# Pooled attention and two MLPs on one core: a reordered end of batch 0, with half weight splits and an earlier third f-block

## What is computed

```python
def _attn_ref(q, k, v):
    k_p = k.reshape(B, H, Sp, 8, D).mean(axis=3)        # Sp = 72 pooled positions
    v_p = v.reshape(B, H, Sp, 8, D).mean(axis=3)
    scores = scale * np.matmul(q, k_p.transpose(0, 1, 3, 2))
    scores = scores - np.max(scores, axis=-1, keepdims=True)
    attn = np.exp(scores)
    attn = attn / (np.sum(attn, axis=-1, keepdims=True) + 1e-09)
    return np.matmul(attn, v_p)

def _moe_ref(x, w_in, w_out):          # x: attention output, heads side by side
    h = np.maximum(x @ w_in, 0.0)
    return h * h @ w_out

def _moe2_ref(x, w_in, w_out):
    h = x @ w_in
    g = np.where(h >= 1, h, np.where(h <= -1, 0.0, (h + 1) ** 2 / 4))
    return g @ w_out
```

## Time and profile before

| | |
|---|---|
| median of 3 runs | 1772.68 us (1771.05 to 1774.06) |
| profiled execution | 1771.15 us |
| its span, first to last instruction | 1769.4 us |
| TensorE busy | 1751.3 us, 99% |
| VectorE, ScalarE, GpSimd busy | 761.8, 553.7, 229.7 us |
| first `output(0)` begins at | 49.12 us |
| mean granted TensorE clock | 0.996 of full speed |

### The profile page before, as it was taken

The page is one execution under the profiler, slowest core; times in us unless marked ns, Lnnn a source line. Parts: engine busy times, 40 slices in busy tenths (PEclk is TensorE's granted clock), DMA queues, the critical chain, the costliest instruction groups (busy, mean ns, idle before and its releaser), DMA issues.

```text
span 1769.4 us, 22412 instructions
## 1 busy us (share of the span) xinstructions
PE 1751.3 (99%) x8371; PEld 1413.9 (80%) x8371; DVE 761.8 (43%) x1211; ACT 553.7 (31%) x970; POOL 229.7 (13%) x254
## 2 busy tenths in 40 slices
PE   8999999999999999999999999999999999999999
PEld 6777777777777777778888788888888888888887
DVE  6664434444444443433235434343434343434343
ACT  5453333333333333332234322222222222222222
POOL 6332313223131231310000000000000000000000
PEclk8999999999999999999999999999999999999999
DMA  6453324242331423213035202020201020201000
GB/s 153 126 153 122 85 71 120 65 124 81 104 99 59 130 74 118 84 61 107 1 116 170 95 1 72 1 71 0 71 0 71 0 71 0 71 0 71 0 24 24
DMA packets 117062, 126.86 MB, mean 72 GB/s; under 512 B 40192, under 2 KB 72448, under 8 KB 116992
## 3 DMA queue, kind: packets, MB, share of 16 engines
q1 hardware_dynamic: 116992, 125.86, 23.1%
HBM read 80.74 MB, written 45.09 MB: 71 GB/s over the span
## 4 chain that ended last, share of the span: by engine, by line
PE 96%; DVE 2%; ACT 1%; issue 0%; DMA 0%; POOL 0%; SPq 0%; ACTq 0%
PE ps_h L931 44%; PE ps_y L968 44%; PE ps_a L882 2%; PE ps_a L906 2%; PE ps_a L919 2%; PE ps_a L896 1%; DVE sq_f L726 1%; DMA first_kv<-in_v 0%; PE ps_h L941 0%; ACT act_f L569 0%; PE ps_y L863 0%; PE ps_y L852 0%; DVE probs L664 0%; DVE stat L662 0%; POOL first_kv L434 0%
## 5 line engine op out<-in xcount | busy, mean ns | idle before, releaser
L931 PE MATMUL ps_h<-xc,w_hi 128*128 128x512 f32 x2288 | 715.1, 394 | 0.0
L931 PEld LDWEIGHTS ps_h<-xc,w_hi 128*128 128x128 f32 x2288 | 423.0, 188 | 93.4 <-issue 9.2
L931 PE MATMUL ps_h<-xc,w_lo 128*128 128x512 f32 x1144 | 446.7, 390 | 0.0
L968 PE MATMUL ps_y<-w_hi,g_hl 128*128 128x512 f32 x1152 | 379.6, 391 | 3.1 <-DVE stage L750 2.2
L968 PE MATMUL ps_y<-g_hl,w_hi 128*128 128x512 f32 x1152 | 366.3, 399 | 1.5 <-DVE g_hl L730 1.5
L726 DVE TENSOR_TENSOR sq_f<-act_f 128x512 f32<-128x512 f32 x144 | 111.4, 774 | 414.0 <-ACT act_f L569 414.0
L968 PEld LDWEIGHTS ps_y<-w_hi,g_hl 128*128 128x128 f32 x1152 | 217.1, 188 | 49.0 <-DVE stage L750 2.6
L968 PEld LDWEIGHTS ps_y<-g_hl,w_hi 128*128 128x128 f32 x1152 | 209.7, 188 | 57.2 <-issue 15.3
L576 ACT ACTIVATE act_f<-act_f,half_bias 128x512 f32<-128x512 f32 x144 | 104.2, 724 | 480.2 <-DVE act_f L737 480.2
L931 PEld LDWEIGHTS ps_h<-xc,w_lo 128*128 128x128 f32 x1144 | 214.5, 188 | 46.4
L968 PE MATMUL ps_y<-g_hl,w_lo 128*128 128x512 f32 x576 | 225.7, 392 | 0.0
(11 more groups left out here) (81 smaller groups left out, 945.9 us busy)
## 6 DMA issues: line engine op xcount, KB each, us to landing
mlp_out_hl<-stage SPq DMA_DIRECT2D x36, 512.0 KB, 4.3
xc<-mlp_out_hl SPq DMA_DIRECT2D x36, 512.0 KB, 5.7
xc<-attn_out_hl SPq DMA_DIRECT2D x32, 512.0 KB, 3.9
attn_out_hl<-xo_hl SPq DMA_DIRECT2D x56, 288.0 KB, 2.3
out<-stage SPq DMA_DIRECT2D x36, 256.0 KB, 2.1
stage<-in_moe_w_in SPq DMA_DIRECT2D x32, 256.0 KB, 3.6
stage<-in_moe_w_out SPq DMA_DIRECT2D x32, 256.0 KB, 4.7
kv_raw<-in_k SPq DMA_DIRECT2D x28, 288.0 KB
```

Of the source, the lines that this page charges most:

```text
L931: mm = nc.tensor.matmul(ps_h[:, f % 2, :], left[:, f, kd * P:(kd + 1) * P], xc[:, buf, right, kd, :], start=(kd == 0 and n == 0), stop=(kd ...
L968: mm = nc.tensor.matmul(ps_y[:, m, :], left, right, start=(f == 0 and n == 0), stop=(f == NF - 1 and n == 2))
```

## The change

Nothing that is computed for the output changes but the place of the factor 1/8 of the mean over v.

- **Large matmuls in front of the value matmuls.** `first_hidden_hi(0)` and `(1)` move ahead of `first_pv(5)` and `first_pv(6)`; the low-weight matmuls of k-blocks 0 and 1 move ahead of `first_pv(7)`. Within a piece the products with x high come first, and the last k-block waits for `x_hi_done` before `x_split`.
- **Half weight splits.** Blocks 0 and 1 are split in halves of 512 columns: ScalarE splits the first halves in units 6 and 7 and the second halves after the last `first_x_hi`; GpSimd makes four half low parts in place of two whole ones. `output(0)` and `output(1)` wait for the second halves. Block 2 is no longer split before the MLP begins: its split on ScalarE and its low part on VectorE stand behind those engines' work on f-blocks 0 and 1.
- **Column-stepped transposes.** `first_turn_p` writes every third column of PSUM, so that `first_copy_p` copies contiguously, with the factor 1/8.
- **A two-tile addition.** Adding 1e-9 was one operation with two constants (add, times 8); it is now the sum of two SBUF tiles, `stat` and `eps_t`.
- **Third f-block at once.** `hidden(2)` of chunk 0 comes before `output(0)`, behind a wait for `relu_done`.
- Also: k is loaded before q, and k is pooled before q is turned for unit 0; GpSimd's sums of v lie more between the scalings; `first_x_lo(4)` to `(7)` all come after `last_scale`; three more matmuls of `keep_warm`.

```diff
@@ SyncE
-                    sp.wait_ge(w_first, n - 3)
+                    sp.wait_ge(w_first, n - 1)
+            first_load_k(0)
             first_load_q(0)
-            first_load_k(0)
@@ GpSimd
-            def first_w_lo(n):
-                pool.wait_ge(w_hi_done, n + 1)
-                nc.gpsimd.tensor_tensor(w_lo[:, n, :], stage[:, n, :], w_hi[:, n, :].bitcast(F32),
+            def first_w_lo(n, half):
+                part = slice(half * DM, (half + 1) * DM)
+                pool.wait_ge(w_first_hi, 2 * half + n + 1)
+                nc.gpsimd.tensor_tensor(w_lo[:, n, part], stage[:, n, part], w_hi[:, n, part].bitcast(F32),
                                         ALU.subtract).then_inc(w_first, 1)
             first_scale(6)
-            first_w_lo(0)
-            first_w_lo(1)
+            for half in range(2):
+                for n in range(2):
+                    first_w_lo(n, half)
@@ ScalarE
+            def first_split_w(n, half):
+                part = slice(half * DM, (half + 1) * DM)
+                act.wait_ge(w_loaded[n], 2 * DMA)
+                nc.scalar.copy(w_hi[:, n, part], stage[:, n, part]).then_inc(w_first_hi, 1)
-                nc.scalar.copy(p_t[:].rearrange("n a (p j) -> n a j p", j=NJ),
-                               ps_y[0:SP_, 0:2, 0:HALF].rearrange("n a (j p) -> n a j p", j=NJ)).then_inc(p_copied, 1)
+                nc.scalar.activation(p_t[:], ps_y[0:SP_, 0:2, 0:HALF], ACT.Copy, scale=1.0 / POOL).then_inc(p_copied, 1)
@@ in chunk(), ScalarE and VectorE
+                    if layer == 1 and c.at(0) and f == 0:
+                        split_w(2)
                     if layer == 1 and c.at(0) and f + 3 < NF:
                         split_w(f + 3)
@@ ScalarE, in the loop over units and behind it
-                if u >= 5:
-                    split_w(u - 5)
+                if u >= NU - 2:
+                    first_split_w(u - NU + 2, 0)
             first_x_hi(NU - 1)
+            for n in range(2):
+                first_split_w(n, 1)
@@ VectorE
-                nc.vector.tensor_scalar(stat[:, u % 2, 2, :], stat[:, u % 2, 1, :], EPS, float(POOL),
-                                        ALU.add, ALU.mult).then_inc(eps_done, 1)
+                nc.vector.tensor_tensor(stat[:, u % 2, 2, :], stat[:, u % 2, 1, :], eps_t[:],
+                                        ALU.add).then_inc(eps_done, 1)
-                if u >= 3:
+                if 3 <= u < NU - 1:
                     first_x_lo(u - 3)
             first_sums(NU - 1)
             last_scale()
-            first_x_lo(NU - 3)
-            first_x_lo(NU - 2)
-            split_w(2)
-            first_x_lo(NU - 1)
+            for u in range(NU - 4, NU):
+                first_x_lo(u)
@@ TensorE
-                        mm = nc.tensor.transpose(ps_y[0:SP_, a, j * QT:(j + 1) * QT],
+                        mm = nc.tensor.transpose(ps_y[0:SP_, a, 0:HALF].rearrange("n (p j) -> n j p", j=NJ)[:, j, :],
+                if c.at(0) and f < 2:
+                    pe.wait_ge(w_first, f + 3)
                 pe.wait_ge(g_ready, c.times(NF, f + 1))
-                    if f + 2 < NF:
+                    if fixed == 0 and f == 0:
+                        pass
+                    elif f + 2 < NF:
...
+            pe.wait_ge(relu_done, 1)
+            hidden(At(0), 0, 2, 0)
             chunk(At(0), 0, True, 1)
```

More of the change, by code:

```diff
@@ L823, in first_turn_q, with first_pool_k @@
                 mm.then_inc(q_turned, 1)
-                if u % 2 == 0:
-                    pe.wait_ge(k_first[u // 2], DMA)
-                    for e in range(POOL):
-                        for a in range(2):
-                            mm = nc.tensor.matmul(first_q_bank(u + 1)[a * D:(a + 1) * D, HALF:HALF + SP_],
-                                                  first_k[:, u // 2, a, e * D:(e + 1) * D], ident[0:SP_, 0:SP_],
-                                                  start=(e == 0), stop=(e == POOL - 1))
-                    mm.then_inc(k_turned, 1)
+            def first_pool_k(hp):
+                pe.wait_ge(k_first[hp], DMA)
+                for e in range(POOL):
+                    for a in range(2):
+                        mm = nc.tensor.matmul(first_q_bank(1)[a * D:(a + 1) * D, HALF:HALF + SP_],
+                                              first_k[:, hp, a, e * D:(e + 1) * D], ident[0:SP_, 0:SP_],
+                                              start=(e == 0), stop=(e == POOL - 1))
+                mm.then_inc(k_turned, 1)
             def first_scores(u):
@@ L934, in hidden, with first_hidden @@
                 mm.then_inc(h_ready, 1)
-            def first_hidden_hi(f, blocks):
-                pe.wait_ge(w_hi_done, f + 1)
-                for kd in blocks:
-                    pe.wait_ge(x_split, 2 * kd + 2)
-                    for right in range(2):
-                        nc.tensor.matmul(ps_h[:, f, :], w_hi[:, f, kd * P:(kd + 1) * P], xc[:, 0, right, kd, :],
-                                         start=(kd == 0 and right == 0), stop=False)
+            def first_hidden(f, left, right, blocks, start=False, stop=False):
+                for kd in blocks:
+                    mm = nc.tensor.matmul(ps_h[:, f, :], left[:, f, kd * P:(kd + 1) * P], xc[:, 0, right, kd, :],
+                                          start=(start and kd == blocks[0]), stop=stop)
+                if stop:
+                    mm.then_inc(h_ready, 1)
+            def first_hidden_hi(f, blocks):
+                pe.wait_ge(w_first_hi, f + 1)
+                pe.wait_ge(x_split, 2 * blocks[-1] + 2)
+                first_hidden(f, w_hi, 0, blocks, start=(0 in blocks))
+                first_hidden(f, w_hi, 1, blocks)
             def first_hidden_lo(f, blocks):
                 pe.wait_ge(w_first, f + 1)
-                for kd in blocks:
-                    mm = nc.tensor.matmul(ps_h[:, f, :], w_lo[:, f, kd * P:(kd + 1) * P], xc[:, 0, 0, kd, :],
-                                          start=False, stop=(kd == KD - 1))
-                if KD - 1 in blocks:
-                    mm.then_inc(h_ready, 1)
+                first_hidden(f, w_lo, 0, blocks)
             def output(c, f, layer):
+                if c.at(0) and f < 2:
+                    pe.wait_ge(w_first, f + 3)
                 pe.wait_ge(g_ready, c.times(NF, f + 1))
@@ L992, in _ @@
             pe.wait_ge(consts_ready, 1)
+            first_pool_k(0)
             first_turn_q(0)
-            keep_warm(2)
+            keep_warm(3)
             first_scores(0)
             first_turn_q(1)
-            keep_warm(1)
+            keep_warm(2)
             for u in range(NU - 1):
@@ L1001, in _ @@
                     first_turn_q(u + 2)
+                if u % 2 == 0 and u + 2 < NU:
+                    first_pool_k(u // 2 + 1)
                 if u < 2:
-                    keep_warm(2)
+                    keep_warm(2 + u)
                 if u >= 2:
```

54 lines of the change are left out of this document (34 added, 20 removed).

## The result

The changed kernel takes 1775.88 us (median of 20 runs, 1772.77 to 1779.11), the kernel before, run beside it, 1771.19 us (20 runs, 1767.01 to 1774.25). The ratio of the runs is 1.0029, with a 95% interval of 1.0021 to 1.0036: slower by 0.29%, some 5 us (4.7 us between the medians). The profiled execution spans 1773.4 us, 4.0 more than before. The time lies in my range, but on its slower side: the forecast "within 0.2%" was wrong. Now and then an execution of any of these kernels runs at a lower clock throughout (1929.57 us in experiment 9, 2179.91 us in experiment 10); the ratios leave such executions out, the medians given for these two experiments take one in each.

A forecast was written before the change was run, and what follows sets the result against it. TensorE was taken as the bound (96% of the chain of waits), with the dense f-block stream's start deciding. Terms -1.8 - 6.6 + 6.3 + 0.85 + 1.8 = +0.55 us gave a median of 1773.2 us, range 1767.5 to 1777.0.

The forecast's parts named there:

- within 0.2%: Whole kernel: a difference under 0.2%, 3.5 us, was to be called no change; this outcome was given 0.54.
- A: Start of batch 0: GpSimd's scaling behind the first v pair alone, k pooled before q; turn at 14.85, -1.8 us.
- B: Last units: shorter splits and copy, large matmuls filling a wait, addition not shut out; first relu at 40.4, -6.6 us.
- R: The start of the first relu, from which the prediction counts times at the start of the MLP.
- C: Start of the MLP: `hidden(2)` waits for block 2's late low part, VectorE taking turns with GpSimd; +6.3 us.
- D: Batch 1's first scores: they follow the turn of q at once and wait for copies of q and k; +0.85 us.
- E: `hidden(2)` and `output(0)`: after TensorE idles about 7.5 us, their first 3.6 us run at half rate; +1.8 us.
- they get in at the next gap: Last units: two-input VectorE operations enter between GpSimd operations, so the addition of unit 7 ends at 33.5.
- third rival: Last units: the two-tile addition waits for both GpSimd half parts, 2.4 us late; sum +2.1, 1774.8 us; chance 0.10.
- second rival: Last units: the clock falls anyway, the path doubles from about 34 on; sum +4.5, 1777.2 us; chance 0.15.
- first rival: Start of the MLP: VectorE largely free of GpSimd, `hidden(2)` wait only +2.6; 1769.6 to 1767.7 us; chance 0.33.
- the sign that I had named for rivals 2 and 3: End of the last units: a first relu after 41 us, where the forecast had it near 38.6.

The follow-up runs named there:

- experiment 9: The kernel before, with GpSimd starting its two whole low weight parts only after VectorE has scaled unit 7: 1770.02 us, ratio 0.9988.
- experiment 10: The changed kernel with GpSimd's order of v sums and scalings as before (both pairs of v summed ahead of the first scaling): 1778.31 us, ratio 1.0036.
- experiment 7: The changed kernel with block 2 split before the MLP, GpSimd's low parts held until VectorE's last scaling, k sums before second half low parts: 1763.35 us, ratio 0.9961.
- Experiment 6: The changed kernel with block 2 split before the MLP and GpSimd's first half low parts held until VectorE's last scaling: 1763.87 us, ratio 0.9965.
- Experiment 4: The changed kernel with GpSimd waiting for VectorE's last scaling before its first half low parts: 1772.27 us, ratio 1.0014.
- Experiment 3: The changed kernel with GpSimd's k sums of batch 1 put before its second half low parts: 1776.08 us, ratio 1.0039.
- experiment 1: The changed kernel with the third f-block, `hidden(2)`, put back behind `output(0)`: 1769.52 us, ratio 1.0000.
- experiment 2: The changed kernel with weight block 2 split before the MLP begins, as before: 1767.12 us, ratio 0.9989.
- experiment 5: The changed kernel with the addition of 1e-9 as one operation with two constants (add, times 1): 1776.14 us, ratio 1.0036.
- experiment 8: The kernel before with only the third f-block at once, `hidden(2)` in front of `output(0)`: 1771.52 us, ratio 0.9999.

## Why the prediction was right, and where wrong

| term | predicted | measured (one profile each) |
|---|---|---|
| A, start of batch 0 | -1.8 | 15.41 - 16.63 = -1.22 |
| B, last units up to R | -6.6 | (42.59 - 47.01) + 1.22 = -3.20 |
| C, from R to the next f-block | +6.3 | 7.88 - 2.11 = +5.77 |
| D, batch 1's first scores | +0.85 | +0.88 |
| E, half clock behind the idle | +1.8 | 12 matmuls in 4.41 us instead of 2.84: +1.57 |
| sum | +0.55 | +3.80, of 4.0 between the spans |

- **The start (A): right in mechanism.** The turn follows the warm matmuls with no idle, and experiment 10 puts 1.09 us on GpSimd's order. The missing 0.6 is no wait: the 32 matmuls that pool k took 1.82 us instead of the 1.2 that I took from the earlier trace rows, since more of them ran at the slower pace of the start (last section). In experiment 7, where they took 1.22 us, the turn comes at 14.74, against my 14.85. The transposes with a step cost nothing, as I had assumed: 0.49 us from the turn to the next product (15.41 to 15.90), before 0.52.
- **The last units (B): the step that failed.** Its sentence was "they get in at the next gap", for the two-tile addition. It did not get in between the two half parts; it waited for both. This is my third rival, to which I gave 0.10, although show the old addition missing just such a gap. I preferred the squares of the earlier trace rows, which do get in, and did not say what tells the two cases apart. The addition makes `first_pv(6)` 1.4 us later than I had it (35.82 + 1.22 against 35.65). Another 2.0 us were lost from there to R: 6.77 us against my 4.75. Experiment 6 takes 5.80 at full clock, with a wait of 0.27 that the changed kernel does not have. So 1.0 to 1.2 is the clock, which fell after the 2.16 us of idle, as my second rival had it but for 3.3 us instead of 10, and 0.8 to 1.0 is that my sum was too short. Experiment 4 prices addition and clock together: 3.24 us from the turn of unit 6 to R.
- **The start of the MLP (C): right.** Order plus turns with GpSimd were both there. Experiment 3 puts the undisturbed start at R + 4.75 (predicted 4.7), contention at 3.1 us; experiments 1 and 2 confirm that the late low part is what TensorE waits for. My first rival, the undisturbed handover, had the largest chance after the forecast (0.33) and is refuted: VectorE's operations took 1.24, 1.64, 1.21 and 0.83 us, where 0.69 is the time alone.
- **Terms D and E: right** within 0.25 us. That the 7.24 us of idle costs the clock again is in the windows (0.60 from 49.1 to 55).
- **The verdict.** The losses (C, D, E: 8.95 predicted, 8.22 measured) were sized well; the gain of B was taken at the favourable end of its range (-7 to -2.5) where the trace held one row for the unfavourable end. With the addition shut out the sum would have been +2.1 (my third rival's), and with the clock's part 3.1 to 3.3 of the measured 4.0. By my own line of 0.2% the outcome is "slower", to which I gave 0.17, and the first relu at 42.59 is the sign that I had named for rivals 2 and 3. That the time lies in the range is in part luck: the range was wide enough for a third rival whose mechanism I held unlikely, and A and B, 4.0 us too favourable, were offset by 0.7 us in C, D and E.

## What to carry to other kernels

When a consumer is moved up, move up its producer, or look up where the producer stands: the same exchange cost 5 us where block 2's low part was made late, and nothing where it was made early. An idle gap in front of TensorE is paid twice where the clock falls after it, and a short operation on the path (six columns wide here) that meets bulk work of GpSimd can open such a gap, here 2.3 us from one of 0.16; holding the bulk work back by one wait was the cheaper order, by 2.7 us. And if a trace shows an operation both missing a gap and getting in, price the miss.

## What the runs showed that I had not expected

- **The start runs at two paces.** The same 32 small matmuls that pool k for unit 0 took 1.22 us in the profile of before, 1.28 in experiment 10, 1.82 in the changed kernel, and in experiment 9 (and 3, 4, 5 and 8) 2.19:

```profile
6.10 2.19 PE L829 MATMUL ps_a<-ident,first_kv 72*64 72x72 f32 x32 [0.15 <-DMA first_kv<-in_k]
```

  With it the turn of unit 0 lies between 14.74 (experiment 7) and 17.3 (3, 4 and 5) for kernels that carry the changed start, and between 16.63 and 18.58 for the old one. The runs of the kernel before and of the changed one spread over 6 to 7 us; how much of that comes from here was not measured. A comparison of absolute times in two profiles would have misled me by 2 us. The Trainium skill ("TensorE: Matmul & The Clock Gate", section "Part 1: The HAM clock gate") says that the number of matmuls at the lower rate when a kernel starts varies from run to run; the trace agrees, with 1.22 to 2.19 us for the same 32. The granted clock of the start reads 1.00 in all these profiles, so here only the durations show it.
- **After the same idle the clock stayed down for different times.** In front of `first_pv(6)` TensorE idles 2.16 us in the changed kernel and 2.18 in experiment 5, with the same instructions around it. The window from 40 to 43.2, changed kernel and experiment 5:

```profile
40.00:43.20 3.20, 3.20 (x14) 2.18 (x12) 0.52 (x2) 2.10 (x5) 1.82 (x2) 0.97 0.09 20
```

```profile
40.00:43.20 3.20, 3.20 (x10) 1.49 (x10) 0.00 (x0) 0.83 (x2) 0.00 (x0) 0.50 0.01 1
```

  In the changed kernel the granted clock is 0.50 for 3.3 us (36.8 to 40.1), and so it is in experiments 1 and 2; R comes 10.6 us behind the turn of unit 6. In experiments 5 and 10 it is 0.50 for about 10 us, though TensorE is busy for nearly all of them, and R comes 13.25 and 13.24 us behind that turn. What decides it stays open. The table of terms is made from an execution of the first kind. Of the changed kernel's 20 runs seven lie apart at 1778.5 to 1779.1 us, the others under 1777.0; the profiled execution of experiment 5 (1778.47 us) lies near the seven. That they are executions of the second kind was not shown.
- **Who gets in at a boundary.** VectorE's addition waited through the boundary between two half low parts of GpSimd, in both forms of it. The squares and remainders behind R got in at one boundary or the next, and in experiment 7 the second square got in between two half low parts too (41.40 to 43.18, while GpSimd took 3.34 us for two that take 2.51 otherwise). So the kind of GpSimd's work does not tell the cases apart; what does was not tried.
